# Reordered attention groups, smaller stores of x between the weight loads, and a new order between the expert layers

## The chip, the cores and the metric

The kernel runs on one core of a Trainium2 chip. The metric is the device time of one launch in microseconds (us), lower is better. A core has five engines with queues of their own: PE (TensorE, matrix products), DVE (VectorE), ACT (ScalarE), POOL (GpSimd) and SP (SyncE, which here only issues DMAs). Each runs its instructions in program order, and they wait for one another through semaphores. Sixteen DMA engines move the data.

## The reference

Attention through 32 memory slots for each head, then a dense gated layer ("MoE 1", one expert), then a routed layer with 8 experts ("MoE 2"), all in float32:

```python
# attention: 8 batches x 8 heads, 576 positions, head size 64, 32 slots
a = softmax(phi, axis=slots)                   # exp, divided by the sum + 1e-9
k_m, v_m = a^T k, a^T v                        # 32 x 64 for each head
x = softmax(q k_m^T / 8) v_m                   # 4608 tokens x 512

# MoE 1: 4608 x 512 -> 2048 -> 512
h = x @ w_in
x2 = (h * sigmoid(1.702 * h)) @ w_out

# MoE 2: each token goes to one of 8 experts, 512 -> 1024 -> 512
e = argmax(x2 @ w_gate)
out = prob[e] * sigmoid(x2 @ w_output_gate)[e] * (relu(x2 @ w1[e]) @ w2[e])
```

## The kernel before

**Attention (stage A).** The 64 heads are worked on in 16 groups of 4 heads (g = 0 to 15, `NG` = 16), two groups to a batch. For each group SP loads phi (288 KB), k and v together (1152 KB) and q (576 KB) into triple buffers (`phT`, `kvm`, `qT`); a load into a buffer waits until the group that used it last has been read. The steps of group g, with the line of the kernel before and its tile:

- DVE takes the maximum of phi (`phi_in`, L1162, `csum<-phT`); ACT the exponential (`exp_phi`, L897, `aT`).
- PE transposes it (`a_transposes`, L636 and L639, `ps<-ident,aT`); ACT copies it to SBUF (`a_out`, L907, `am`).
- PE forms k_m and v_m (L653 and L658, `ps<-kvm,am`); ACT scales them with the inverse sums (`kv_scale`, L916, `kvs`); POOL lays v_m out in blocks (`v_blocks`, L1584, `vbd`).
- PE transposes k_m (L668), ACT copies it (`k_out`, L923, `kmT`), and PE forms the scores (L681, `ps<-qT,kmT`).
- DVE transposes the scores (L1173), takes the row maxima (L1175) and subtracts them (L1177, `sc<-sc,scs`); ACT takes the exponential (`exp_scores`, L901); DVE sums and inverts (`inverses`, L1184, L1188, L1190); POOL multiplies by the inverse (`normalize`, L1576); DVE transposes back (`attn_out`, L1196, `pT`).
- PE multiplies by v_m in two halves (`out_half`, L628, `ps<-pT,vbd`); ACT copies the halves out (`x_out`, L933) into `keep` (batches 0 to 6) or `xo` (batch 7).

These steps are staggered by hand: while PE has group g, the scores of g-1 and the outputs of g-3 are worked on. `group(g)` of each engine's program writes that order out; nothing reorders it. `warm_up` (L691) is a product of zeros that nothing reads.

**MoE 1 (stage B).** x is handled in 9 tiles of 512 tokens, each number split into a high and a low part (`xs`: high by a cast, low by a subtraction), so that each float32 product is made of three fast ones. A tile has 16 steps f: `mm1` (L717, 12 matmuls, x by w_in), the gate `g_step` on ACT and DVE (sigmoid L988, product L1237, high part L992, low part L1239), then `mm2` (L750, 12 matmuls, by w_out). In the first tile the weights come too: SP loads 32 chunks of 256 KB (four of them during the attention) (`load_w`) into four raw buffers, and POOL splits each into high and low (`split_w` L1555 and L1557, `split_w_in` L1564 and L1566), which `mm1` and `mm2` wait for through `s_wlo`. W shares memory with `keep`, so POOL may write its second half (steps f = 8 to 15 of w_in and of w_out) only after the x kept there is stored to DRAM (`store_kept`, `kept_stored`). The first tile's first steps are written between the last attention products by hand:

```python
            out_half(NG - 3, 0)
            mm1(0, 0)
            out_half(NG - 3, 1)
            out_half(NG - 2, 0)
            mm1(0, 1)
            out_half(NG - 2, 1)
            for i in range(2):
                out_half(NG - 1, i, (6, 4)[i])
            mm1(0, 2)
```

**MoE 2 (stage C).** Records of 128 tokens (blocks i) are loaded in the order of experts. PE does `block_h` (L791, `ps<-W,cx`) and `block_y` (L820, `ps<-W,chT`), two blocks apart; `dve_x_t`, `act_x_hi` and `dve_x_lo` prepare a block's x (`cxT`, `cx`), `act_relu` and `dve_relu` the two halves of the hidden layer, `act_h_move` moves it with four DMAs, and `dve_h_t`, `act_h_hi` and `dve_h_lo` (L1361, L1053, L1374) transpose and split it (`chT`). Between the stages lie the transposition of the last tile (L849), its logits (L760), the routing of its tokens (`route1`, `route2`) and the tables of blocks on DVE. Six blocks (0 to 5) are written out by hand before the loop starts.

## Time and profile before

| what | value |
|---|---|
| time, three runs | 1333.48 us median (1333.1 to 1334.02) |
| the profiled execution | 1334.72 us, span 1333.0 us |
| PE busy | 1309.6 us, 98% of the span |
| DVE, ACT, POOL busy | 629.7, 388.3, 548.4 us |
| granted PE clock, mean | 0.995 of full |
| DMA share, each 10 us from 10 to 120 us | 0.94 to 1.03 of the time of 16 engines |

The span is the time from the first instruction to the last of one core in one profiled execution; the execution's own time has 1.72 us more around it. An engine is busy while an instruction of it runs; a group's idle time is what the engine stood still just before it, with what ended the wait.

### The profile page before, as it was taken

Reading aid. Unit: us, or ns where it says so; the run is one execution under the profiler, and the core shown is the slowest. Engines: PE = TensorE matmul, PEld = TensorE weight load, DVE = VectorE, ACT = ScalarE, POOL = GpSimd, SP = SyncE. Lnnn points to the kernel's source line nnn. Section 1 sums busy time; section 2 is a strip of 40 time slices with the busy share of each in tenths; the row PEclk is TensorE's granted clock in tenths of the full one; section 3 lists DMA queues with packets and bytes.
Section 4 is the critical chain, followed back from the end, with each engine's and each line's share of the span. In section 5 each row is a group of like instructions: output and inputs, shape, how many; then the busy total and the mean of one; then the engine's idle time right before and its main releaser. Section 6 shows DMA issues by size and latency. Waiting matters only on the chain.

```text
span 1333.0 us, 23549 instructions
## 1 busy us (share of the span) xinstructions
PE 1309.6 (98%) x6872; PEld 1053.5 (79%) x6873; DVE 629.7 (47%) x1291; ACT 388.3 (29%) x725; POOL 548.4 (41%) x649
## 2 busy tenths in 40 slices
PE   7999999999999999999999999999999999999998
PEld 3447888888888888888888888887788888888886
DVE  5893343434433434334434344347555555555553
ACT  4663232222222322222222222223322222222221
POOL 2567944444433434334334343412443242433332
PEclk8999999999999999999999999999999999999999
DMA  9997456575465554654655646647873789549882
GB/s 380 416 405 278 127 201 192 194 194 199 159 180 194 166 178 169 189 174 172 179 185 174 180 170 184 199 159 232 256 206 101 221 238 258 166 128 257 249 247 71
DMA packets 153418, 274.18 MB, mean 206 GB/s; under 512 B 17363, under 2 KB 54612, under 8 KB 150804
## 3 DMA queue, kind: packets, MB, share of 16 engines
q1 hardware_dynamic: 96676, 203.21, 45.2%
q10 hardware_dynamic: 43728, 38.55, 11.8%
q0 software_dynamic: 12960, 31.72, 7.7%
q8 instruction: 31, 0.51, 0.2%
q14 instruction: 23, 0.19, 0.0%
HBM read 144.92 MB, written 100.45 MB: 184 GB/s over the span
## 4 chain that ended last, share of the span: by engine, by line
PE 92%; DVE 3%; DMA 2%; issue 1%; ACT 1%; ACTq 0%; POOL 0%; SPq 0%; POOLq 0%
PE ps L717 29%; PE ps L750 29%; PE ps L820 16%; PE ps L791 15%; DMA phT<-in_phi 2%; PE ps L760 1%; PE ps L628 1%; DVE sc L1173 1%; DVE scs L1175 1%; DVE scs L1184 0%; PE ps L681 0%; ACTq L1046 0%; PE ps L653 0%; DVE sc L1177 0%; DMA cq<-ch 0%
## 5 line engine op out<-in xcount | busy, mean ns | idle before, releaser
L717 PE MATMUL ps<-xs,W 128*128 (+1 forms) x1728 | 417.5, 390 | 0.0
L750 PE MATMUL ps<-W,gs 128*128 128x512 f32 x1728 | 415.0, 389 | 0.1
L717 PEld LDWEIGHTS ps<-xs,W 128*128 128x128 f32 x1728 | 322.9, 188 | 69.7 <-issue 3.1
L750 PEld LDWEIGHTS ps<-W,gs 128*128 128x128 f32 x1728 | 324.2, 188 | 67.8 <-DVE gs L1239 0.5
L1237 DVE TENSOR_TENSOR gate<-ps,gate 128x512 f32<-128x512 f32 x144 | 99.5, 691 | 369.9 <-ACT gate L988 369.9
L988 ACT ACTIVATE gate<-ps 128x512 f32<-128x512 f32 x144 | 86.1, 598 | 467.8 <-PE ps L717 467.3
L820 PE MATMUL ps<-W,chT 128*128 (+1 forms) x936 | 218.3, 389 | 1.5 <-DVE chT L1374 1.5
L791 PE MATMUL ps<-W,cx 128*128 (+1 forms) x936 | 218.5, 389 | 0.4 <-issue 0.4
L1617 POOL CAST whi<-raw 128x512 fp32r<-128x512 f32 x128 | 83.1, 649 | 328.2 <-DMA raw<-in_moe_w 328.2
L820 PEld LDWEIGHTS ps<-W,chT 128*128 128x128 f32 x936 | 175.6, 188 | 38.8 <-issue 2.3
L791 PEld LDWEIGHTS ps<-W,cx 128*128 128x128 f32 x936 | 175.5, 188 | 37.3 <-issue 1.0
L1619 POOL TENSOR_TENSOR raw<-raw,whi 128x512 f32<-128x512 f32 x128 | 171.7, 1341 | 22.4 <-POOL whi L1617 21.1
L383 POOL DMA_DIRECT2D crec<-record_scratch x160 | 90.0, 563 | 187.3 <-DMA out<-cy,cmeta 117.1
L1239 DVE TENSOR_TENSOR gs<-gate,gs 128x512 fp32r<-128x512 f32 x144 | 117.5, 816 | 99.7 <-ACT gs L992 99.7
L992 ACT CAST gs<-gate 128x512 fp32r<-128x512 f32 x144 | 89.4, 621 | 111.3 <-DVE gate L1237 109.1
L1053 ACT CAST chT<-cqT 128x512 fp32r<-128x512 f32 x41 | 25.2, 620 | 201.2 <-issue 152.8
L1625 POOL DMA_INDIRECT record_scratch<-rec,posi x36 | 36.0, 1000 | 99.8 <-DVE posi L1303 90.5
L1676 POOL DMA_INDIRECT out<-cy,cmeta x39 | 42.0, 1078 | 76.2 <-ACT cy L1061 69.0
L1338 DVE TENSOR_TENSOR cx<-cxT,cx 128x512 fp32r<-128x512 f32 x40 | 43.6, 1090 | 58.5 <-ACT cx L1021 56.8
L1374 DVE TENSOR_TENSOR chT<-cqT,chT 128x512 fp32r<-128x512 f32 x78 | 53.2, 691 | 38.0 <-ACT chT L1053 36.7
L1352 DVE TENSOR_SCALAR ch<-ps 128x512 f32<-128x512 f32 x37 | 25.5, 690 | 68.0 <-PE ps L791 67.8
L1361 DVE STREAM_TRANSPOSE cqT<-cq 128x512 f32<-128x512 f32 x78 | 50.6, 686 | 12.6 <-DMA cq<-ch 10.8
(159 smaller groups left out, 779.9 us busy)
## 6 DMA issues: line engine op xcount, KB each, us to landing
W<-expert_scratch SPq DMA_DIRECT2D x24, 2048.0 KB, 11.2
raw<-in_moe_w SPq DMA_DIRECT2D x128, 256.0 KB, 2.8
expert_scratch<-whi SPq DMA_DIRECT2D x128, 256.0 KB, 2.7
expert_scratch<-raw SPq DMA_DIRECT2D x128, 256.0 KB, 3.0
cq<-ch ACTq DMA_DIRECT2D x156, 128.0 KB, 3.8
kvm<-in_kv SPq DMA_DIRECT2D x15, 1152.0 KB, 9.9
crec<-record_scratch POOLq DMA_DIRECT2D x160, 64.0 KB, 3.4
qT<-in_q SPq DMA_DIRECT2D x16, 576.0 KB, 8.2
```

The lines of the kernel that those rows point to most:

```text
L383: eng.dma_start(crec[b * M:(b + 1) * M, r % 3], rows[:, b * P:(b + 1) * P].rearrange("(h n) d -> n h d", n=M)).then_inc(loaded, 16)
L717: mm = pe.matmul(ps[:, f % 2, :], W[:, col:col + P], xs[:, bass.ds(x0 + (x_lo * K1 + c) * T, T)], start=(c == 0 and w_lo + x_lo == 0), sto ...
L750: mm = pe.matmul(ps[:, 2 + s, :], gs[:, f % 2, g_lo, s * P:(s + 1) * P], w_out_sb[:, f, w_lo, :], start=(f == 0 and g_lo + w_lo == 0), sto ...
L791: mm = pe.matmul(ps[:, 3 * u + j, :], cx[:, u, x_lo, c, :], W[:, bass.ds(col, 512)], start=(c == 0 and x_lo + w_lo == 0), stop=(c == K1 - ...
L820: mm = pe.matmul(ps[:, 5 + r % 2, :], chT[:, r % 2, h_lo, c, :], W[:, bass.ds(col, DM)], start=(c == 0 and h_lo + w_lo == 0), stop=(c == C ...
L988: act.activation(gate[:, f % 2, :], ps[:, f % 2, :], ACT.Sigmoid, scale=QTOK).then_inc(b_sig, 1)
L992: act.copy(gs[:, f % 2, 0, :], gate[:, f % 2, :]).then_inc(b_ghi, 1)
L1237: dve.tensor_tensor(gate[:, f % 2, :], ps[:, f % 2, :], gate[:, f % 2, :], ALU.mult).then_inc(b_g, 1)
L1239: dve.tensor_tensor(gs[:, f % 2, 1, :], gate[:, f % 2, :], gs[:, f % 2, 0, :].bitcast(F32), ALU.subtract).then_inc(b_glo, 1)
L1374: dve.tensor_tensor(by_h(1, j), cqT[:, j * 512:(j + 1) * 512].rearrange("p (h c n) -> p h c n", h=2, n=M), by_h(0, j).bitcast(F32), ALU.su ...
L1617: pool.tensor_copy(whi[:, u, :], raw[:, u, :]).then_inc(e_hi, 1)
L1619: pool.tensor_tensor(raw[:, u, :], raw[:, u, :], whi[:, u, :].bitcast(F32), ALU.subtract).then_inc(e_lo, 1)
```

## The change

It has three parts.

1. Attention. The subtraction of the row maxima moves from DVE to POOL for groups 0 to 14 (`less_max`). phi is loaded, and its maximum and exponential are taken, one group earlier. On PE the transposition of phi for the next group moves behind that of k, in two parts, the k/v product goes to another PSUM bank, and two more warm-up products stand before group 0. ACT's order in a group changes. At the end of the stage a first sigmoid stands ahead of the last exponential of the scores, POOL makes both parts of the first two pieces of x, one more `mm1` comes ahead of the first `mm2`, and splits of weights come in another order.
2. Stores of x. In place of two stores of five batches and two for each of batches 5 and 6, the first half of the features of batches 0 to 4 is stored in one piece, and all else in pieces of 576 KB, each after one load of a weight chunk. POOL waits for the first half of the features only before w_in's steps 8 to 11, and for the rest before steps 12 to 15 and w_out's steps 8 and on.
3. Between the expert layers. PE has the transposition of the last x2 tile between the two halves of `block_h` for block 0. DVE has `route1` ahead of `dve_x_lo(2, 0)`, and `dve_x_t(3, 3)` ahead of two `dve_scale`, and `dve_relu(3, 1)` ahead of `dve_x_t(5, 5)`. ACT has `act_x_hi(3, 1)` ahead of `act_y(1, 1)`. Two casts (the high part of block 5's x and of block 3's hidden layer) move from ACT to DVE. POOL loads block 6's records ahead of `scatter_out(1, 1)`.

The core of the diff:

```diff
@@ SP, loads of the attention
             load_phi(0)
             sp.dma_start(ident[:], cst["ident"]).then_inc(s_cst, 16)
+            load_phi(1)
             load_q(0)
+            load_phi(2)
             for g in range(1, NG):
-                load_phi(g)
                 load_kv(g)
                 load_q(g)
+                if g + 2 < NG:
+                    load_phi(g + 2)
@@ SP, first tile (load_w_out(f), load_w_in(c, k): one chunk each)
-            for c in range(2):
-                load_w(K1 + 2 * c, w_out_v[c])
-                load_w(K1 + 2 * c + 1, w_in_part(c, 1))
-            store_kept(0, FIRST, s_xfirst)
+            load_w_out(0)
+            load_w_out(1)
+            load_w_in(0, 1)
+            load_w_in(1, 1)
+            store_kept(0, FIRST, 0, s_xu0)
...
+                    load_w_in(2, 1)
+                    store_kept(FIRST, 1, 0, s_xu0)
+                    load_w_in(3, 1)
+                    store_kept(FIRST + 1, 1, 0, s_xu0)
+                    load_w_out(2)
+                    store_kept(0, 1, 1, s_x10)
+                    load_w_out(3)
+                    store_kept(1, 1, 1, s_x11)
+                    load_w_out(4)
...
@@ PE
+            def group(g):
+                kv_product(g)
+                if g >= 3:
+                    out_half(g - 3, 0)
+                k_transposes(g)
+                if g + 1 < NG:
+                    a_main(g + 1)
+                    pe.wait_ge(s_kmT, g + 1)
+                    a_rest(g + 1)
+                scores(g)
                 if g >= 3:
                     out_half(g - 3, 1)
...
             out_half(NG - 3, 0)
             mm1(0, 0)
             out_half(NG - 3, 1)
+            mm1(0, 1)
             out_half(NG - 2, 0)
-            mm1(0, 1)
             out_half(NG - 2, 1)
+            mm1(0, 2)
             for i in range(2):
                 out_half(NG - 1, i, (6, 4)[i])
-            mm1(0, 2)
+            mm1(0, 3)
...
-            for j in range(2):
-                block_h_half(0, j, 0, 0)
+            block_h_half(0, 0, 0, 0)
             last_x2_transpose(NT - 1)
+            block_h_half(0, 1, 0, 0)
             last_logits(NT - 1)
@@ ACT, group(g)
+                kv_scale(g, u)
                 if g >= 4:
                     x_out(g - 4, 1)
+                k_out(g)
+                if g == 0:
+                    exp_phi(1)
+                if g >= 3:
+                    x_out(g - 3, 0)
+                if g + 1 < NG:
+                    a_out(g + 1)
                 if g:
                     exp_scores(g - 1, 1 - u)
+                if g + 2 < NG:
+                    exp_phi(g + 2)
@@ ACT, first tile
                     if first and f == 2:
-                        stage_a_done(act)
+                        act.wait_ge(s_xst, 16)
@@ DVE, group(g)
-                if g + 1 < NG:
-                    phi_in(g + 1)
-                inverses(g, u, g >= 2, True)
-                if g:
-                    less_max(g - 1, 1 - u)
+                scores_in(g - 1, (g - 1) % 2)
+                inverses(g - 2 if g >= 2 else None, g + 1 if g + 1 < NG else None)
+                scores_max(g - 1, (g - 1) % 2)
+                if g + 2 < NG:
+                    phi_in(g + 2)
                 if g >= 2:
                     attn_out(g - 2)
@@ DVE, blocks 3 to 5
+            dve_x_t(3, 3)
             dve_scale(1, 1)
             dve_scale(2, 2)
-            dve_x_t(3, 3)
...
+            dve_relu(3, 1)
             dve_x_t(5, 5)
-            dve_relu(3, 1)
-
+            dve_x_hi(5, 1)
             dve_x_lo(5, 1)
             dve_scale(5, 5)
             dve_relu(4, 0)
             dve_h_t(3, 1)
+            dve_h_hi(3, 1)
             dve_h_lo(3, 1)
@@ POOL
             for g in range(NG):
+                if g - 1 in QUARTER:
+                    c = QUARTER.index(g - 1)
+                    split_w_in(c, c, 0)
+                if g >= NG - 2:
+                    x_first(g - (NG - 2))
                 if g >= 2:
                     normalize(g - 2, g % 2)
+                if g:
+                    less_max(g - 1, 1 - g % 2)
                 v_blocks(g, g % 4)
...
+            split_w(n_out(0), 0)
+            normalize(NG - 2, 0)
```

**PE, from the start of the program to the k/v product of group 1.** L691 and L744 are the warm-up, `ident,aT` the transposition of phi, `kvm,am` the k/v product, `ident,kvs` the transposition of k, `qT,kmT` the scores. Before:

```order
L691 MATMUL ps<-padrec 128x512
L653 MATMUL ps<-kvm,am 32x128 x16
L658 MATMUL ps<-kvm,am 32x128 x4
L636 MATMUL ps<-ident,aT 128x128 x4
L639 MATMUL ps<-ident,aT 64x64 x2
L668 MATMUL ps<-ident,kvs 64x128 x2
L681 MATMUL ps<-qT,kmT 32x288 x8
L653 MATMUL ps<-kvm,am 32x128 x16
```

Now:

```order
L744 MATMUL ps<-padrec 128x512 x3
L695 MATMUL ps<-kvm,am 32x128 x16
L700 MATMUL ps<-kvm,am 32x128 x4
L709 MATMUL ps<-ident,kvs 64x128 x2
L723 MATMUL ps<-qT,kmT 32x288 x8
L676 MATMUL ps<-ident,aT 128x128 x4
L682 MATMUL ps<-ident,aT 64x64 x2
L695 MATMUL ps<-kvm,am 32x128 x16
```

Two warm-up products are added, and group 1's transposition has moved from before group 0's scores to behind them.

**DVE, one group in the middle of the attention.** `csum<-phT` is the maximum of phi, `sc<-ps` the transposition of the scores, `scs<-sc` a row sum or a row maximum, `pT<-sc` the transposition back. Before:

```order
L1162 TENSOR_REDUCE csum<-phT 128x1
L1184 TENSOR_REDUCE scs<-sc 128x18
L1188 TENSOR_SCALAR scs<-scs 128x19
L1190 RECIPROCAL scs<-scs 128x19
L1173 STREAM_TRANSPOSE sc<-ps 128x288 x2
L1175 TENSOR_REDUCE scs<-sc 128x18
L1177 TENSOR_TENSOR sc<-sc,scs 128x576
L1196 STREAM_TRANSPOSE pT<-sc 128x576
```

Now:

```order
L1247 STREAM_TRANSPOSE sc<-ps 128x288 x2
L1261 TENSOR_REDUCE scs<-sc 128x18
L1265 TENSOR_SCALAR scs<-scs 128x19
L1267 RECIPROCAL scs<-scs 128x19
L1252 TENSOR_REDUCE scs<-sc 128x18
L1236 TENSOR_REDUCE csum<-phT 128x1
L1274 STREAM_TRANSPOSE pT<-sc 128x576
```

The subtraction is gone, and the transposition of the scores stands first.

**ACT, from the last copies of kept x to the store of the last x.** `gate<-ps` is the sigmoid, `sc<-sc` the exponential of the last group's scores, `gs<-gate` the high part of the gate. Before:

```order
L901 ACTIVATE sc<-sc 128x576
L933 COPY keep<-ps 128x2x288
L933 COPY xo<-ps 128x2x288
L988 ACT_TABLE_LOAD
L988 ACTIVATE gate<-ps 128x512
L992 CAST gs<-gate 128x512
L933 COPY xo<-ps 128x2x288 x3
L938 DMA xT_scratch<-xo 128x4x576
```

Now:

```order
L1048 ACT_TABLE_LOAD
L1048 ACTIVATE gate<-ps 128x512
L962 ACT_TABLE_LOAD
L962 ACTIVATE sc<-sc 128x576
L994 COPY keep<-ps 128x2x288
L1055 CAST gs<-gate 128x512
L1048 ACT_TABLE_LOAD
L1048 ACTIVATE gate<-ps 128x512
L994 COPY xo<-ps 128x2x288 x2
L1055 CAST gs<-gate 128x512
L994 COPY xo<-ps 128x2x288 x2
L999 DMA xT_scratch<-xo 128x4x576
```

The exponential now stands between two sigmoids, and each change of function has a table load of its own: three in place of one.

## Rows read from the trace of the kernel before

**Rows 1.** Page, part 1: busy time of each engine, share of the span, instructions

```profile
PE 1309.6 (98%) x6872; PEld 1053.5 (79%) x6873; DVE 629.7 (47%) x1291; ACT 388.3 (29%) x725; POOL 548.4 (41%) x649
```

**Rows 2.** Windows: length, busy time of PE, PEld, DVE, ACT, POOL, clock, DMA, GB/s

```profile
79.54:84.44 4.90, 4.68 (x79) 2.57 (x77) 4.76 (x10) 3.58 (x9) 2.12 (x2) 1.00 1.02 419
93.42:96.83 3.41, 3.36 (x24) 1.42 (x25) 3.31 (x7) 1.17 (x2) 1.61 (x3) 0.50 0.99 419
120.00:140.00 20.00, 20.00 (x90) 16.56 (x89) 6.57 (x8) 4.26 (x7) 19.20 (x20) 1.00 0.43 121
```

**Rows 3.** Timeline of SP and DMA issues of 76.0 to 79.3 us (last column: landing)

```profile
76.15 0.33 SPq L457 DMA_DIRECT2D kvm<-in_kv  x1
...
kvm<-in_kv SPq DMA_DIRECT2D x1, 1152.0 KB, 9.4
qT<-in_q SPq DMA_DIRECT2D x1, 576.0 KB, 7.9
```

**Rows 4.** Timeline of PE, start: start, length, engine, line, operation, count

```profile
9.79 2.07 PE L691 MATMUL ps<-padrec 128*128 128x512 f32 x2
11.79 1.94 PE L653 MATMUL ps<-kvm,am 128*32 128x128 f32 x32
...
25.32 1.08 PE L653 MATMUL ps<-kvm,am 128*32 128x128 f32 x32
```

**Rows 5.** Timelines of DVE and POOL: the subtraction, and POOL's operation of that shape

```profile
81.42 0.76 DVE L1177 TENSOR_TENSOR sc<-sc,scs 128x576 f32<-128x576 f32 x1
...
84.87 1.16 POOL L1576 TENSOR_TENSOR sc<-sc,scs 128x576 f32<-128x576 f32 x1 [2.38 <-DVE scs L1190]
```

**Rows 6.** Timeline of PE, end of the attention

```profile
89.33 1.08 PE L653 MATMUL ps<-kvm,am 128*32 128x128 f32 x32
...
91.54 0.44 PE L668 MATMUL ps<-ident,kvs 128*64 128x128 f32 x4 [0.77 <-ACT kvs L916]
...
93.47 1.21 PE L681 MATMUL ps<-qT,kmT 64*32 64x288 f32 x16 [0.80 <-ACT kmT L923]
94.61 2.29 PE L628 MATMUL ps<-pT,vbd 64*128 64x288 f32 x8
96.83 3.03 PE L717 MATMUL ps<-xs,W 128*128 128x512 f32 x12
99.79 1.24 PE L628 MATMUL ps<-pT,vbd 64*128 64x288 f32 x8
...
105.65 0.76 PE L628 MATMUL ps<-pT,vbd 64*128 64x288 f32 x4 [0.51 <-ACT xo L933]
...
109.20 5.60 PE L750 MATMUL ps<-W,gs 128*128 128x512 f32 x24
```

**Rows 7.** Timeline of ACT, the table load and the first sigmoid

```profile
101.13 0.65 ACT L933 COPY xo<-ps 128x576 f32<-128x576 f32 x1
101.79 1.28 ACT L988 ACT_TABLE_LOAD   x1
103.09 0.60 ACT L988 ACTIVATE gate<-ps 128x512 f32<-128x512 f32 x1
```

**Rows 8.** Timeline of DVE, a small operation beside POOL's subtractions of 87.35 to 89.86

```profile
88.61 1.28 DVE L1188 TENSOR_SCALAR scs<-scs 128x19 f32<-128x19 f32 x1
```

**Rows 9.** Timeline of POOL, the wait in the first tile's splits

```profile
119.87 1.11 POOL L1555 CAST W<-raw 128x512 fp32r<-128x512 f32 x1 [4.46 <-DMA raw<-in_moe_w_out]
```

**Rows 10.** Timeline of PE, idle times between the expert layers

```profile
904.63 1.08 PE L760 MATMUL ps<-x2x,wg 128*32 128x128 f32 x32 [0.83 <-ACT x2x L1103]
...
923.28 11.22 PE L820 MATMUL ps<-W,chT 128*128 128x512 f32 x48 [0.80 <-DVE chT L1374]
934.92 16.60 PE L791 MATMUL ps<-W,cx 128*128 x72 [0.42 <-issue]
952.25 5.72 PE L820 MATMUL ps<-W,chT 128*128 x24 [0.73 <-DVE chT L1374]
```

**Rows 11.** Timeline of DVE, transposition of block 5's x

```profile
941.14 0.71 DVE L1333 STREAM_TRANSPOSE cxT<-crec 128x512 f32<-128x512 f32 x1 [2.70 <-DMA cmeta<-record_scratch]
```

More of the change, by code:

```diff
@@ new lines, in sp_tile @@
+                    sp.dma_start(stage[0], cst["before"]).then_inc(s_cst2, 16)
+                    sp.dma_start(stage[1], gates).then_inc(s_cst2, 16)
+                    sp.wait_ge(b_setup, 1)
+                    sp.dma_start(padrec[:].bitcast(I32)[:, DM + NE + 1:DM + NE + 2], cst["padtoken"]).then_inc(b_cst, 16)
+                    load_w_out(8)
+                    load_w_out(9)
+                    for c in range(K1):
+                        load_w_in(c, 3)
+                    for f in range(10, C1):
+                        load_w_out(f)
@@ L695, in _ @@
             pe.wait_ge(s_cst, 16)
-            a_transposes(0)
-            warm_up(1)
-            for g in range(NG):
+            a_main(0)
+            a_rest(0)
+            warm_up(3)
+            kv_product(0)
+            k_transposes(0)
+            scores(0)
+            a_main(1)
+            a_rest(1)
+            for g in range(1, NG):
                 group(g)
@@ L825, in pe_tile @@
                 for f in range(STEPS):
-                    if not first or f >= 3:
+                    if not first or f >= 4:
                         mm1(t, f)
-                    if f:
+                    if first and f == 4:
+                        mm2(t, f - 2)
+                    if f and not (first and f == 3):
                         mm2(t, f - 1)
-                    elif not first:
+                    if f == 0 and not first:
                         mm2(t - 1, C1 - 1)
@@ L1073, in act_tile @@
                         load_x(t + 1)
-                    if not first or f:
+                    if not first or f >= 2:
                         g_step(t, f)
                     if first and f == 2:
-                        stage_a_done(act)
+                        act.wait_ge(s_xst, 16)
+                    if first and f == STEPS - 1:
+                        kept_stored(act)
                     if not first:
@@ L1088, in act_tile @@
                         x_hi(t + 1, f - 11)
-            g_step(0, 0)
-            x_out(NG - 2, 1)
-            x_out(NG - 1, 0, 6)
-            x_out(NG - 1, 1, 4)
+            g_sigmoid(0, 0)
+            exp_scores(NG - 1, 1)
+            x_out(NG - 3, 1)
+            g_hi(0, 0)
+            g_sigmoid(0, 1)
+            for i in range(2):
+                x_out(NG - 2, i)
+            g_hi(0, 1)
+            for i in range(2):
+                x_out(NG - 1, i, (6, 4)[i])
             store_last()
```

265 lines of the change are left out of this document (149 added, 116 removed).

## The prediction

> **What bounds the kernel now.** I read the page first. PE is busy for 1309.6 of 1333.0 us [rows 1]: the products of the three stages stand on it almost without a gap, and nothing in the change removes a product. Time can only come from PE's idle time and from the attention, where PE's instructions wait for others or run below their best. So I went on with the windows of the attention, and with the timeline of PE wherever idle time stands before a row.
>
> In the attention's second half one group takes 4.9 us. In a window of that length DVE is busy for 4.76 of 4.90 us, PE for 4.68, ACT for 3.58, POOL for 2.12, and the DMA engines all the time at 419 GB/s [rows 2]. Two bounds lie on top of each other: DVE's work for a group, and the 2016 KB that a group loads (2.06 MB by 0.42 MB/us is 4.9 us). Which came last is seen in the last group: its k and v were issued at 76.15 and landed 9.4 us later, at 85.6 [rows 3], but PE began their product only at 89.33 [rows 6]. The compute engines are 3.8 us behind the data. That lag can be won; the landing itself can't, since the bytes up to it are the same in both kernels.
>
> Behind that product PE does what is left of the attention and three `mm1` until 109.20, and from there it has no idle time of over 0.12 us until 904 us (the timeline shows none). In these 19.9 us it is idle for 0.77, 0.80 and 0.51 us, and it runs at half clock from 93.42 to 96.83 (granted 0.50, its lower level of 1.2 GHz), after the two idle times; four halves of attention output take 2.29 us there against 1.24 us later [rows 2, 6]. Between the expert layers four idle times stand ahead of PE's products: 0.83, 0.80, 0.42 and 0.73 us, together 2.8 us [rows 10].
>
> **The attention's pace.** The subtraction leaves DVE, 0.76 us [rows 5], so that DVE needs 4.76 - 0.76 = 4.0 us for a group. POOL takes it at the 1.16 us of its own operation of that shape [rows 5]: 2.12 + 1.16 = 3.3 us, and 5.3 us in the four groups in which it also splits a chunk (0.61 and some 1.3 us). These fall into the 1.8 us in which POOL would wait for the inverse sums, so at most 0.5 us of each shows. PE has 4.68 us in a group, less than the loads' 4.9. Its new order leaves the same instructions, and each wait has cover: `kmT`'s copy lies behind the main transposition of phi, `kvs` behind half an output. ACT's 3.58 us are unchanged. So the loads alone set the pace, and compute may run at 4.7 us for as long as it is behind them.
>
> **The start is worse.** The two added warm-up products run at half clock, the first takes 2.07 us and about 1.7 us without its start [rows 4]; they put off the product of group 0 from 11.79 by 3.4 us, which gives 1.0 us back as it then runs at full clock (1.94 against 1.08 us [rows 4]). Group 1's transposition and copy now lie behind the scores of group 0, another 1.4 us. So the compute starts 3.5 to 4 us late: group 3's product moves from 25.32 [rows 4] to about 29. At 4.7 us for each of the next 12 groups the last group's product could begin at 29 + 56 = 85. The loads feel the start too. phi of group 4, which stands ahead of group 3's k and v on SP, waits for the exponential of group 1, which on ACT now stands behind group 0's copy of k, at about 19 us; the loads issued earlier have landed at 19.3, and a load needs about 2 us to begin. That is up to 1.5 us without a transfer, and nothing makes it up in a stage bound by the loads. I take 0.8 us of it, as the present kernel's k and v of group 3 landed late too. The last product then begins at 85.6 + 0.8 + 0.1 = 86.5 in place of 89.33: **2.8 us won**. Bounds: 85.7 (nothing lost) and 89 (the pace is 4.9 to 5.0 us, since PE's waits aren't all covered).
>
> **The tail.** From that product to 109.20 PE needs 19.9 us, less 2.1 us of idle time and 1.5 us of half clock, so 16.3 us of dense work [rows 6]. It now has a fourth `mm1` ahead of the first `mm2`, the same work in another place, 2.7 us; the corresponding point of the kernel before is 109.20 + 2.7 = 111.9. Still idle will be about 0.4 us before the last scores, whose copy of k has no other work over it. Walking the new order through with X as the last product's start: the last scores end at X + 3.6, the first `mm1` runs from X + 5.0 to 7.7. Then ACT loads the sigmoid's table ahead of time, does the sigmoid (X + 8.4), loads the exponential's table (1.28 us [rows 7]), and does the exponential (X + 10.4). DVE sums, inverts, multiplies (0.8 to 1.6 us) and transposes: `pT` of the last group is there at X + 14.1 to 15.5. PE asks for it at X + 14.9, behind the third `mm1`. The third load, 1.28 us, lies ahead of the sigmoid for the fourth `mm1`, whose own wait (for DVE's product of step 1) ends at X + 15.4 to 16.4, against a need at X + 16.1. Both are near a stall; I allow 0.4 us. So the corresponding point is X + 16.3 + 2.7 + 0.8 = X + 19.8 = 106.3 against 111.9: 5.6 us, of which **2.8 us are the tail's**.
>
> In rows 7 the table load takes 1.28 us, begins when the copy before it has ended (101.13 + 0.65), and the sigmoid follows it at once. The Trainium skill (ScalarE: Activation LUTs, What ACT_TABLE_LOAD costs) puts a change of set at about 2.66 us, a load of 1.28 and a drain of 1.38. No drain is seen in rows 7, so the trace doesn't agree; by that rule the last `pT` would come 1.4 us later. What a stall there would cost is the third rival below.
>
> A small DVE operation can also be held up by POOL: the one at 88.61 took 1.28 us until POOL's second subtraction ended, and 0.17 us elsewhere [rows 8]. In the tail POOL splits without a pause, and DVE's sums with 1e-9 and inversions stand in the chain to `pT`; that is the upper end of X + 15.5. The Trainium skill (SBUF — State Buffer, Who interferes with whom) says the same of this operation and excludes reductions; the steady groups keep theirs, so their pace stands.
>
> **Stores and weights.** The four chunks of w_in for steps 4 to 7 are wanted at about X + 24, earlier than now by 5.6 us. POOL splits a chunk in 2.0 us (19.20 us busy for 10 in 20 us [rows 2]). It ends w_out 0 and the fourth of them, six chunks and a `normalize`, at about X + 18.7, if they have landed. The big store of 2880 KB is 7 us of transfers, the two pieces of 576 KB 1.4 us each; the last of the four chunks lands at about X + 14. The cover is 5 us. POOL waits 4.46 us for a store and a chunk at 119.87 now [rows 9] and PE feels nothing; the new pieces come no later. Cost: 0. If the cover is gone, each microsecond of delay is one of the whole.
>
> **Between the layers.** The 0.83 us before the logits is the wait for copies of the transposed tile; the second half of block 0 now covers it, and all of routing comes 0.8 us earlier. The 0.80 us at 923.28 comes from block 1's four moves on ACT and stays. The 0.42 us before block 3 waits for its low part on DVE; `dve_x_t(3, 3)` goes ahead of six small operations, 0.9 us: gone. The 0.73 us before block 3's second product comes from DVE's half of its relu, queued behind a transposition that waited 2.70 us for block 5's records until 941.14 [rows 11]; it now stands ahead, and the casts take 1.1 and 0.7 us on DVE, which has that much idle time there. Gone too. **2.0 us won**, between 0.8 (only the logits) and 2.8.
>
> **Sum.** 2.8 + 2.8 + 2.0 = 7.6 us. Against the profiled execution (span 1333.0, time 1334.72) that is a span of 1325.4 and a time of 1327.1; that execution lies 1.2 us above the median, so against 1333.48 the time is 1325.9 us.
>
> **Rivals.**
> - *The attention's pace doesn't change* (12%). PE's chain of waits, not DVE, would set it. For it speaks that PE is busy for 4.68 of 4.90 us. The 12 groups from 25.32 to 89.33 took 5.33 us each now; the late start then moves X to 29 + 64 = 93, and the end by 93 + 19.8 - 111.9 = +0.9, less 2.0: 1332.4, no change. Against it: DVE shows no idle time in these groups, PE does.
> - *The pace improves by half* (15%): X = 89, time 1328.4.
> - *The tail stalls on the last exponential* (10%). With 1.4 us more on each switch and POOL's hold on DVE, PE waits 2 to 3 us before the last outputs: 1328 to 1329.
> - *Slower* (4%): the first tile's weights. POOL has 1.16 us more in each group and casts two pieces of x; its last `normalize` and w_in's chunks, loaded only after earlier ones are split, come late, and step 4 waits. It decides from where the last chunk is split 5.5 + 7.6 = 13 us later than I work out: at X + 32 it gives 1333.5, at X + 36 1337.5. Against it: POOL's present pace.
> - The forecast, 1323.5 to 1327.5: 59%.
>
> Faster by over 0.2% (2.7 us, about what a measurement of this kernel can tell) is below 1330.8: 0.87. Within it: 0.09. Slower: 0.04. The range goes from 1323.0 (nothing lost at the start, 2.8 us between the layers) to 1329.5, which takes in the half-improved pace and the stalled tail.
>
> **What would show it.** The last k/v product at 86 to 87 us, not 89.3; the pace of DVE below 4.2 us busy in a group; three table loads of 1.28 us, with less than 1 us idle before the last outputs; no idle time on PE from then to the logits; idle times of 0.83, 0.42 and 0.73 us gone and that of 0.80 us kept. Wrong would be: k/v products that follow one another by more than 4.9 us where no chunk is loaded, a DMA share well under 1 from 19 to 25 us, or a wait of step 4 for W.

## The result, and the profile after

The changed kernel takes 1329.81 us (median of 12 runs, 1328.08 to 1331.56) against 1333.1 us for the kernel before beside it (12 runs, 1332.13 to 1334.56); the ratio is 0.9972, with a 95% interval of 0.9965 to 0.9979. A repeat of the comparison gave 1329.18 us and 0.9966 (0.9954 to 0.9979). So it is faster, by 3.3 to 3.8 us; the forecast was 7.6 us, and its time, 1325.9 us, lies 3.9 us below the median; the upper end of its range, 1329.5 us, lies between the two medians. Why only half of it came is what the rest is about.

Page of the changed kernel, one line of part 1 (busy time) and one of part 4 (the chain that ended last):

```profile
PE 1306.9 (98%) x6876; PEld 1052.2 (79%) x6877; DVE 624.0 (47%) x1281; ACT 389.5 (29%) x722; POOL 564.8 (43%) x666
...
PE 93%; DMA 4%; DVE 1%; ACT 1%; issue 0%; POOL 0%; ACTq 0%; SPq 0%; POOLq 0%; DVEq 0%
```

The two profiled executions, cut at the same events of PE (in us; each mark is the start of a PE row; the fourth `mm1` is ahead of the mark of the tail only after the change, so its 2.72 us are added to 109.20 before):

| stretch | before | after | won | forecast |
|---|---|---|---|---|
| start to the last k/v product | 89.33 | 86.59 | 2.74 | 2.8 |
| to the first `mm2` (before: and one `mm1`) | 22.59 | 20.79 | 1.80 | 2.8 |
| to block 0 of the expert layers | 784.53 | 784.53 | 0.00 | 0 |
| to block 3's second product | 55.80 | 54.45 | 1.35 | 2.0 |
| to the end of the span | 380.73 | 380.67 | 0.06 | 0 |

The sum is 5.95 us of span (1332.98 less 1327.03). The medians differ by only 3.3: the profiled execution of before took 1334.72 us, 1.6 above the median of its 12 runs, and that of after 1328.66, 1.2 below its own. A term read from one pair of executions can be far off: the tail's 1.80 becomes 0.25 beside another execution of the old attention (experiment 1).

**The attention.** Windows of the changed kernel (columns as in rows 2), a group of the second half and the start:

```profile
10.00:20.00 10.00, 8.21 (x114) 4.19 (x113) 2.25 (x8) 3.24 (x8) 0.45 (x1) 0.91 1.02 423
...
77.16:81.99 4.83, 4.67 (x76) 2.56 (x76) 3.93 (x9) 3.63 (x9) 3.32 (x5) 1.00 1.03 425
```

Beside the window 79.54:84.44 of [rows 2], DVE has 3.93 us of work in place of 4.76, POOL 3.32 in place of 2.12. The DMA share never falls, at the start either. Timeline of PE after, to be read against [rows 6]:

```profile
77.16 1.08 PE L695 MATMUL ps<-kvm,am 128*32 128x128 f32 x32 [0.21 <-DMA kvm<-in_kv]
...
81.99 1.08 PE L695 MATMUL ps<-kvm,am 128*32 128x128 f32 x32 [0.16 <-DMA kvm<-in_kv]
...
86.59 1.08 PE L695 MATMUL ps<-kvm,am 128*32 128x128 f32 x32
...
89.44 0.72 PE L723 MATMUL ps<-qT,kmT 64*32 64x288 f32 x16 [0.36 <-ACT kmT L984]
...
91.41 0.96 PE L776 MATMUL ps<-xs,W 128*128 128x512 f32 x3
```

The k/v product's releaser is now the load itself. In groups 6 to 14 (from 41.10 us on) it begins 0.04 or 0.05 us after its k and v have landed, where before it began 3.7 to 4.8 us after. The last group is an exception: its k and v landed at 86.14, and PE, which from 81.99 on shows no idle time, came to their product 0.45 us later.

**The tail.** PE, and under it DVE, of the changed kernel:

```profile
102.37 1.24 PE L668 MATMUL ps<-pT,vbd 64*128 64x288 f32 x8 [0.16 <-DVE pT L1274]
104.52 3.02 PE L776 MATMUL ps<-xs,W 128*128 128x512 f32 x12 [0.91 <-DVE gate L1306]
107.38 0.84 PE L808 MATMUL ps<-W,gs 128*128 128x512 f32 x3
```

```profile
101.53 0.78 DVE L1274 STREAM_TRANSPOSE pT<-sc 128x576 f32<-128x576 f32 x1
102.24 1.63 DVE L1311 TENSOR_TENSOR gs<-gate,gs 128x512 fp32r<-128x512 f32 x1
103.79 0.68 DVE L1306 TENSOR_TENSOR gate<-ps,gate 128x512 f32<-128x512 f32 x1
```

The 0.91 us before the fourth `mm1` are new. It waits for DVE's product of step 1 (L1306), which stands behind the low part of step 0 (L1311); that one took 1.63 us, and 0.69 us where POOL left it alone. ACT's tables, in the same execution:

```profile
92.78 1.28 ACT L1048 ACT_TABLE_LOAD   x1
94.48 0.60 ACT L1048 ACTIVATE gate<-ps 128x512 f32<-128x512 f32 x1 [0.42 <-PE ps L776]
95.10 1.28 ACT L962 ACT_TABLE_LOAD   x1
96.39 0.69 ACT L962 ACTIVATE sc<-sc 128x576 f32<-128x576 f32 x1
...
99.11 1.28 ACT L1048 ACT_TABLE_LOAD   x1
100.41 0.60 ACT L1048 ACTIVATE gate<-ps 128x512 f32<-128x512 f32 x1
```

Each load takes 1.28 us. The second and the third begin 0.02 us after the instruction before them has ended, and the function follows at once; behind the first, the sigmoid waits 0.42 us for PE's product. So the trace agrees with the load that the Trainium skill states (ScalarE: Activation LUTs, What ACT_TABLE_LOAD costs), and not with the drain that it adds.

**The weights.** The longest wait of POOL's splits for a chunk before 125 us, at [rows 9]'s place (a second one, 0.95 us, stands at 122.65):

```profile
117.22 0.61 POOL L1656 CAST W<-raw 128x512 fp32r<-128x512 f32 x1 [2.88 <-DMA raw<-in_moe_w_out]
```

PE has no idle time of over 0.12 us from 107.38 to 904 us.

**Between the layers.** PE, and under it ACT and DVE, of the changed kernel, against [rows 10]:

```profile
903.18 8.45 PE L849 MATMUL ps<-W,cx 128*128 128x512 f32 x36
...
918.50 11.15 PE L878 MATMUL ps<-W,chT 128*128 128x512 f32 x48 [1.43 <-DVE chT L1473]
929.92 16.60 PE L849 MATMUL ps<-W,cx 128*128 x72 [0.27 <-issue]
946.36 4.01 PE L878 MATMUL ps<-W,chT 128*128 x17
```

```profile
913.12 3.18 ACTq L1113 DMA_DIRECT2D cq<-ch  x4
916.34 1.14 ACT L1120 CAST chT<-cqT 128x512 fp32r<-128x512 f32 x2 [3.29 <-issue]
```

```profile
917.06 1.29 DVE L1473 TENSOR_TENSOR chT<-cqT,chT 128x512 fp32r<-128x512 f32 x2 [1.37 <-ACT chT L1120]
```

The 0.83 and 0.73 us are gone, 0.42 has become 0.27, and 0.80 has grown to 1.43. What stands ahead of block 3's low part on DVE is now the transposition of its x, and that waits for the block's records:

```profile
926.75 0.71 DVE L1426 STREAM_TRANSPOSE cxT<-crec 128x512 f32<-128x512 f32 x1 [0.63 <-DMA cmeta<-record_scratch]
```

### The profile page after: what moved, and what is told of

Read it like the earlier page. It is cut to its first block, busy times and chain, and to the rows that moved or that the text cites. A ratio compares the mean times of both kernels' runs of the same rounds, so it can differ in the third digit from the quotient of the medians.

```text
span 1327.0 us, 23583 instructions
## 1 busy us (share of the span) xinstructions
PE 1306.9 (98%) x6876; PEld 1052.2 (79%) x6877; DVE 624.0 (47%) x1281; ACT 389.5 (29%) x722; POOL 564.8 (43%) x666
## 4 chain that ended last, share of the span: by engine, by line
PE 93%; DMA 4%; DVE 1%; ACT 1%; issue 0%; POOL 0%; ACTq 0%; SPq 0%; POOLq 0%; DVEq 0%
PE ps L808 29%; PE ps L776 29%; PE ps L849 16%; PE ps L878 16%; DMA kvm<-in_kv 3%; PE ps L818 1%; PE ps L695 1%; DMA phT<-in_phi 0%; PE ps L676 0%; PE ps L744 0%; PE ps L668 0%; ACTq L1113 0%; POOL sc L1677 0%; ACT aT L958 0%; PE ps L709 0%
## 5 line engine op out<-in xcount | busy, mean ns | idle before, releaser
L1306 DVE TENSOR_TENSOR gate<-ps,gate 128x512 f32<-128x512 f32 x144 | 99.6, 692 | 361.7 <-ACT gate L1048 361.4
L1311 DVE TENSOR_TENSOR gs<-gate,gs 128x512 fp32r<-128x512 f32 x144 | 117.1, 813 | 102.0 <-ACT gs L1055 102.0
```

The costliest lines, as they stand in the source:

```text
L1306: dve.tensor_tensor(gate[:, f % 2, :], ps[:, f % 2, :], gate[:, f % 2, :], ALU.mult).then_inc(b_g, 1)
L1311: dve.tensor_tensor(gs[:, f % 2, 1, :], gate[:, f % 2, :], gs[:, f % 2, 0, :].bitcast(F32), ALU.subtract).then_inc(b_glo, 1)
```

## The experiments

Each is the kernel named, with the edit shown. "Pace" is the distance of two k/v products, X the start of the last one. The time is the median, the ratio that to the kernel before beside it, with its 95% interval. Where a profiled execution is compared, it is one execution.

**1. The last part alone** (before, with the new order between the expert layers). Edit, at its core:

```diff
@@ PE, DVE, ACT, POOL of stages B and C: as part 3 of the change
-            for j in range(2):
-                block_h_half(0, j, 0, 0)
+            block_h_half(0, 0, 0, 0)
             last_x2_transpose(NT - 1)
+            block_h_half(0, 1, 0, 0)
...
+            dve_x_t(3, 3)
             dve_scale(1, 1)
             dve_scale(2, 2)
-            dve_x_t(3, 3)
...
```

> The kernel before with the third part alone (order and casts between the expert layers). By the two profiles the stretch from block 0's product to block 3's second product is 1.35 us shorter: theory A expects 1.0 to 1.5 us less than the kernel before, with the idle times of 0.83 and 0.73 us gone and that before block 1's second product kept at 0.8. My prediction had 2.0. Rival: the gap before block 1's second product grows as in the changed kernel (1.43), as it is caused by routing coming earlier; then 0.7 us.

Measured: 1331.03 us (11 runs), ratio 0.9990 (0.9981 to 0.9999). From block 0 to block 3's second product 54.18 us against 55.80: 1.6 won, by the ratio 1.3. Here too the 0.80 us grew, to 1.48, as the rival said; the other three idle times are gone. This kernel has the attention of before untouched, so its profile is a second execution of it. PE, timeline, to be laid beside [rows 6]:

```profile
89.08 1.08 PE L653 MATMUL ps<-kvm,am 128*32 128x128 f32 x32
...
93.22 0.72 PE L681 MATMUL ps<-qT,kmT 64*32 64x288 f32 x16 [0.80 <-ACT kmT L923]
93.86 1.24 PE L628 MATMUL ps<-pT,vbd 64*128 64x288 f32 x8
95.04 1.20 PE L717 MATMUL ps<-xs,W 128*128 128x512 f32 x4
```

The idle times of 0.77 and 0.80 us are the same, but the half clock behind them is not there: the outputs take 1.24 us, not 2.29, and from X to the first `mm1` are 5.96 us, not 7.50. The 1.5 us of half clock belong to the one execution that was profiled before: the kernel before with smaller loads (experiment 4) has the same idle times too, and 5.96 us as well. From X to the end of the tail this execution needs 21.04 us (18.32 and one `mm1`), the changed kernel 20.79: by this pair the new order of the tail wins 0.25 us, not 2.8.

The same profile shows what holds the old attention. Issues of SP from 73.5 to 77 us with their time to landing, and the timeline of SP and of DVE:

```profile
phT<-in_phi SPq DMA_DIRECT2D x1, 288.0 KB, 8.3
...
74.28 0.43 SPq L452 DMA_DIRECT2D phT<-in_phi  x1
...
82.62 0.75 DVE L1160 TENSOR_REDUCE csum<-phT 128x1 f32<-128x576 f32 x1
```

phi of the last group, issued at 74.28, lands 8.3 us later, at 82.6; DVE's maximum of it begins at 82.62, and the product 6.46 us behind that.

**2. The subtraction back on DVE** (after, without `less_max` on POOL):

```diff
@@ DVE, group(g), behind scores_max
+                dve.wait_ge(s_dv, DVE_A * g)
+                dve.tensor_tensor(by_m((g - 1) % 2), by_m((g - 1) % 2), each_m((g - 1) % 2, 0), ALU.subtract).then_inc(s_mx, 1)
@@ POOL
-                if g:
-                    less_max(g - 1, 1 - g % 2)
```

> The changed kernel with the subtraction of the maxima back on DVE for all groups. Theory D (DVE's relief is what lets compute follow the loads): DVE has 4.8 us per group again, the last k/v product comes 2 to 3 us later, the time is 2 to 3 us longer than the changed kernel's. Rival (the new order of PE, ACT and of phi is what won): DVE's 4.8 us are still under the loads' 4.9, the last product stays within 0.5 us of 86.6, and the time within 0.7 us. As the lag at the start is 3 us at group 3, and the loads give 0.1 us per group and 0.6 us per weight chunk, I expect the last product at 87 to 88, and 1 us longer.

Measured: 1333.71 us (11 runs), ratio 1.0005 (0.9996 to 1.0014), 4.5 us above the changed kernel and all of the gain lost, more than either theory had. X is 90.62. DVE and PE in one group:

```profile
79.47 1.21 DVE L1287 TENSOR_TENSOR sc<-sc,scs 128x576 f32<-128x576 f32 x1
80.60 0.74 DVE L1236 TENSOR_REDUCE csum<-phT 128x1 f32<-128x576 f32 x1
81.27 0.76 DVE L1274 STREAM_TRANSPOSE pT<-sc 128x576 f32<-128x576 f32 x1
```

```profile
82.08 0.76 PE L668 MATMUL ps<-pT,vbd 64*128 64x288 f32 x4 [0.64 <-DVE pT L1274]
```

The subtraction costs 1.21 us there (0.76 in [rows 5]), DVE is busy for 5.09 us of each 5.30, and PE waits 0.64 us for `pT` in each group. The new order alone is worse than the old.

**3. The subtraction on POOL, in the old order** (before, plus `less_max` on POOL for all groups but the last, nothing else; the function itself is left out here).

```diff
@@ DVE
-                wait(dve, s_dv, DVE_A * g + 3)
-                dve.tensor_tensor(by_m(u), by_m(u), each_m(u, 0), ALU.subtract).then_inc(s_mx, 1)
+                if g == NG - 1:
+                    wait(dve, s_dv, DVE_A * g + 3)
+                    dve.tensor_tensor(by_m(u), by_m(u), each_m(u, 0), ALU.subtract).then_inc(s_mx, 1)
@@ POOL, behind normalize(g - 2, g % 2)
+                if g:
+                    less_max(g - 1, 1 - g % 2)
```

> The kernel before with one edit: POOL takes the subtraction of the maxima of every group but the last, and nothing else changes (order of PE and ACT as before). If DVE's load alone had set the old pace (4.74 of 4.88 us busy), the last k/v product comes as in the changed kernel, at 85.5 to 87 us, and the time falls by 2 to 3 us. If the old order's chain of waits sets it (the exponential now comes 0.4 us later behind POOL's slower operation, and on ACT and PE the next group stands behind it), the product stays at 88.5 to 90 and the time within 0.1%. I lean to the second, 60 to 40: so the new order and the new engine each do nothing alone.

Measured: 1332.72 us (11 runs), ratio 0.9999 (0.9990 to 1.0008); X is 89.51. DVE has 4.08 us of work in a group now, 0.7 less than before, and nothing is won. Window of one group, DVE and PE:

```profile
79.94:84.68 4.74, 4.67 (x78) 2.56 (x76) 4.08 (x9) 3.58 (x9) 2.73 (x4) 1.00 1.01 417
```

```profile
77.52 0.75 DVE L1162 TENSOR_REDUCE csum<-phT 128x1 f32<-128x576 f32 x1 [0.39 <-DMA phT<-in_phi]
```

```profile
89.51 1.08 PE L653 MATMUL ps<-kvm,am 128*32 128x128 f32 x32
```

With less to do DVE only waits, for phi. The last product comes 7.1 us after phi's landing in place of 6.5, and no group from 4 on takes less than 6.9: POOL's subtraction in the chain takes 1.16 us where DVE's took 0.76. So neither the new engine nor the new order wins alone; only together do they. Which parts of the new order are needed (phi's earlier load, PE's order, ACT's) was not tried one by one.

**4. Fewer bytes** (q loaded by half from group 3 on, so half of the scores' operand is stale: the output, and the experts' load with it, differ; only the attention is read). In the changed kernel and in the kernel before:

```diff
+                part = QA * D if g < 3 else QA * D // 2
-                sp.dma_start(qT[g % 3][:].rearrange("p c h n -> p (c h n)"), q[g * P:(g + 1) * P, :]).then_inc(s_q[g % 3], 16)
+                sp.dma_start(qT[g % 3][:].rearrange("p c h n -> p (c h n)")[:, 0:part], q[g * P:(g + 1) * P, 0:part]).then_inc(s_q[g % 3], 16)
```

> The changed kernel with only half of q loaded from group 3 on; the other half of the buffer keeps older numbers, so the scores are others. 288 KB less in each of 13 groups, 0.7 us of transfers each. Theory L (in the changed kernel the loads set the pace from group 6 on, each k/v product begins 0.05 us after its landing): the groups now follow one another by the compute's own 4.6 us, and the last product begins at 82 to 83 us in place of 86.6 to 87.2. Rival (another engine is as slow): it moves by less than 1 us.

> The kernel before with the same smaller loads. Its k/v products begin 3.8 us after the landing, so by theory L the loads don't set its pace but DVE's chain does: the groups that now take 4.9 us stay at 4.9, only the four with a weight chunk (5.5 us) may fall to 4.9. The last product moves from 89.1 to no less than 86.5. Rival (the loads are the bound in both): it moves as in the changed kernel, by over 4 us.

Measured, one execution each. Changed kernel: X at 83.98, 2.6 and 3.2 us earlier than in the two profiles of it. Kernel before: X at 84.95, 4.1 to 4.4 earlier. A window of one group of each, the changed kernel first:

```profile
74.78:79.38 4.60, 4.60 (x78) 2.56 (x77) 4.27 (x9) 3.83 (x9) 2.87 (x5) 1.00 0.95 382
```

```profile
75.35:80.12 4.77, 4.67 (x78) 2.56 (x76) 4.63 (x10) 3.58 (x9) 2.00 (x2) 1.00 0.91 360
```

Both kernels were paced by the loads: the old one moved as the rival said, past the 86.5 that I had set as its limit. Freed of them the new order makes a group in 4.60 us, with PE never idle, and the old one in 4.77. There DVE is behind the loads in the old order: its maximum of phi begins 2.0 and 2.1 us after phi has landed in the last two groups.

**5. One warm-up product** (after).

```diff
-            warm_up(3)
+            warm_up(1)
```

> The changed kernel with one warm-up product before group 0 in place of three. The prediction said that the two added ones put off group 0 and starve the loads by up to 1.5 us. In the profile the loads never stood still (phi of group 4 was issued at 17.0, the load before it landed at 19.3). Theory A: group 0's product begins 1.5 to 2 us earlier, the last one at the same time, since the loads set it: time the same within 0.5 us. Rival 1 (the start costs): 1 us faster. Rival 2 (the warm-ups keep the clock up): without them the clock is 0.5 for one or two more stretches of 3.4 us, the groups run slower there, and the time is the same or up to 1 us longer.

Measured: 1328.75 us (5 runs), ratio 0.9965 (0.9952 to 0.9979). Group 0's product comes at 11.94 in place of 13.50; X does not move. PE at X:

```profile
87.11 1.08 PE L695 MATMUL ps<-kvm,am 128*32 128x128 f32 x32 [1.12 <-DMA kvm<-in_kv]
```

What the start gains, the loads take. In this execution the last k and v landed at 87.06 (86.14 in the first one). The landing moves between executions: in four of the eight profiles with the changed attention and all its loads (the two of the changed kernel and those of experiments 9 and 10) it comes 4.2 us after the one before, in the other four (experiments 5 to 8) 5.7 to 5.8 us after, and PE then waits 1.0 to 1.1 us at X. The order and the times of issue don't make the difference: in experiments 5 and 10 the load was issued at 73.00 and 73.01, the next q landed at 88.35 in both, and k and v landed at 87.06 and 85.38.

**6. The gate's product first** (after; DVE's product of step 1 ahead of the low part of step 0).

```diff
+            g_product(0, 1)
             g_lo(0, 0)
+            g_lo(0, 1)
...
-                    if not first or f:
+                    if not first or f >= 2:
```

> The changed kernel with DVE's product of step 1 ahead of the low part of step 0. In both profiles of the changed kernel PE is idle for 0.91 us before the fourth mm1 and waits for that product, which DVE does behind a low part of 1.63 us. Theory T (this one wait is what the tail lost): the 0.9 us are gone, the first mm2 begins 0.9 us earlier in relation to the last k/v product (20.8 to 19.9 us), the time is 0.9 us shorter. Rival: the low part, now later, holds up the first mm2, and the idle time only moves there.

Measured: 1328.0 us (5 runs), ratio 0.9961 (0.9948 to 0.9975). From the first `mm1` to the first `mm2` 14.74 us against 15.97 and 15.98 in the two profiles of the changed kernel. That overstates it: in experiment 5, without this edit, the same stretch took 14.85. There PE had waited 1.12 us for the last k and v, as it did for 1.09 us here, and DVE had caught up; in experiments 7 and 8, with the same wait, the stretch is 15.10 and 14.99 and the idle time before the fourth `mm1` 0.28 and 0.18 us. So its 0.91 us stand only in executions in which the load doesn't make PE wait at X; the two take each other's place. This run therefore doesn't show what the edit wins; the profile of experiment 10 does.

**7. Block 1's cast on DVE** (after).

```diff
@@ ACT
-            act_h_hi(1, 1)
@@ DVE
+            dve_h_hi(1, 1)
```

> The changed kernel with the high part of block 1's hidden layer cast on DVE, which on ACT stands behind the issue of block 2's four moves. Theory C (PE reaches block 1's second product 0.9 us earlier than before, but that cast stays where it was, so the idle time of 0.8 us grew to 1.1 to 1.4): the idle time before that product is gone; as the tables behind it on DVE come only some 0.6 us earlier, PE's idle time before block 3 grows from 0.3 to 0.5 us to about 1.0; net 0.5 to 0.9 us faster. Rival: what holds it is the landing of block 1's moves, and DVE's cast changes nothing.

Measured: 1329.03 us (5 runs), ratio 0.9966 (0.9952 to 0.9979); block 0 to block 3's second product 54.02 us (54.45 and 54.38 before the edit). PE still waits 1.04 us before block 1's second product, and none before block 3: both parts of theory C failed. DVE there:

```profile
914.65 1.30 DVE L1459 STREAM_TRANSPOSE cqT<-cq 128x512 f32<-128x512 f32 x2 [0.87 <-DVE crec L1568]
915.88 0.46 DVE L1571 TENSOR_REDUCE crec<-crec 1x43 f32<-1x344 f32 x1
916.26 0.49 DVE L1572 TENSOR_REDUCE crec<-crec 1x43 f32<-1x344 f32 x1
916.78 0.76 DVE L1465 CAST chT<-cqT 128x512 fp32r<-128x512 f32 x2
```

The cast no longer waits for ACT's four moves, but two reductions of the block tables now stand ahead of it: one wait took the place of the other.

**8. The stores first** (after; the second half of the features of batches 0 to 4 stored right behind the big store, ahead of the weights of steps 4 to 7 in part and of all later ones).

```diff
@@ SP, behind store_kept(0, FIRST, 0, s_xu0)
+            for b, stored in enumerate((s_x10, s_x11, s_xu1, s_xu1, s_xu1)):
+                store_kept(b, 1, 1, stored)
... (and the five taken out at their old places)
```

> The changed kernel with the five single pieces of x (batches 0 to 4) stored right behind the big store in place of between the loads of W. If the weights of steps 4 to 7 have some 5 us of cover, the 2.9 MB, up to 7 us of transfers ahead of W's chunks, show as POOL's waits and at most 2 us of PE's idle time before 140 us: time +0 to +2 us. If the rival is right that the first tile hangs on the weights, every microsecond shows: +4 to +7 us. I expect +0 to +2.

Measured: 1328.28 us (6 runs), ratio 0.9966 (0.9954 to 0.9978). 2.9 MB now stand ahead of these weights; POOL waits for a chunk at 105.73 us, PE for none, and the time is no longer than the changed kernel's:

```profile
105.73 0.61 POOL L1665 CAST W<-raw 128x512 fp32r<-128x512 f32 x1 [2.88 <-DMA raw<-in_moe_w_in]
```

**9. One table load** (after; ACT's last exponential ahead of the first sigmoid).

```diff
+            exp_scores(NG - 1, 1)
             g_sigmoid(0, 0)
-            exp_scores(NG - 1, 1)
```

> The changed kernel with ACT's last exponential ahead of the first sigmoid, so that ACT changes its table once in place of three times. If the table loads (1.28 us each) held the tail, the last outputs' waits go and the time falls by up to 1 us. If DVE's order before the fourth mm1 holds it, the sigmoid that comes later puts off DVE's products and so that mm1: 0 to +1.5 us. I expect the second.

Measured: 1329.49 us (6 runs), ratio 0.9970 (0.9958 to 0.9982): no difference from the changed kernel. ACT:

```profile
95.76 0.69 ACT L962 ACTIVATE sc<-sc 128x576 f32<-128x576 f32 x1 [3.31 <-DVE sc L1321]
96.46 1.28 ACT L1048 ACT_TABLE_LOAD   x1
```

Two loads (2.56 us) are saved, and ACT waits 3.31 us for DVE's subtraction instead. The order written with three loads costs nothing that these runs show.

**10. Experiments 5, 6 and 7 together.** The edit is the three above.

> The changed kernel with three edits: DVE makes the gate product of step 1 ahead of the low part of step 0, block 1's high cast is on DVE, one warm-up product in place of three. If the idle time before the fourth mm1 (0.91 us) and half of the gap before block 1's second product are what was given back, the time is 1.2 to 1.8 us below the changed kernel's 1329.2 to 1329.8: 1327.4 to 1328.4. If these only shift which wait comes last, it is 1328.5 to 1329.5.

Measured: 1327.89 us (5 runs, 1326.6 to 1329.48), ratio 0.9962 (0.9948 to 0.9975). It is the lowest median, 1.3 to 1.9 us below those of the changed kernel, though the intervals of the ratios overlap, and experiment 6 alone had 1328.0: what the other two edits add doesn't show. PE and DVE in the tail:

```profile
101.61 1.24 PE L668 MATMUL ps<-pT,vbd 64*128 64x288 f32 x8 [0.17 <-DVE pT L1273]
102.78 3.04 PE L776 MATMUL ps<-xs,W 128*128 128x512 f32 x12
105.66 0.62 PE L808 MATMUL ps<-W,gs 128*128 128x512 f32 x2
```

```profile
101.48 0.65 DVE L1305 TENSOR_TENSOR gate<-ps,gate 128x512 f32<-128x512 f32 x1
102.05 2.08 DVE L1310 TENSOR_TENSOR gs<-gate,gs 128x512 fp32r<-128x512 f32 x2
```

Here PE had not waited at X (85.83), as in the changed kernel's profile; an idle time of 0.17 us before the outputs is there as well, and the 0.91 us before the fourth `mm1` are gone. First `mm1` to first `mm2`: 15.02 against 15.97. Block 1's gap stays at 1.05 us.

The changed kernel unaltered, the repeat named at the top, had this expectation:

> The changed kernel once more, for a second profile. In the first one its span was 6.0 us shorter than that of the kernel before, while the medians differ by 3.3 us. Theory A (the shown profile is a lucky one): this profile has a span of 1328 to 1329 us, and the last k/v product or the point where PE becomes dense comes 1 to 2 us later than 86.6 and 107.4. Theory B (the time is lost outside the span): the span is again 1327 and the time still 1329.8.

Measured, besides the times at the top: the profiled execution has a span of 1327.5 us, X is 87.16 and the first `mm2` comes at 107.94, 0.6 us later than in the first profile. That is less than theory A had. Theory B fails too: outside the span are 1.7 us, as in the other two profiles. The larger part of what the two first profiles show too much lies in the one of the kernel before, 1.6 us above its median.

## Why the prediction was half right

**The last k/v product: near in its time, wrong in its reason.** Forecast 86.5, measured 86.59 and 87.16, and 85.83 to 88.38 in the six other profiles with this attention and all its loads; that the first came so near is in part luck. The landing moved by 0.6 us to 86.14 (forecast 0.8), and the start, warm-ups and all, cost nothing that the loads didn't cover (experiment 5). "The compute engines are 3.8 us behind the data" was so; that DVE's 4.76 us of work kept them there was not. Experiment 3 takes 0.7 us of work in each group from DVE and X stays. In the kernel before, DVE's maximum begins 0.02 us after phi has landed in nearly every group, and the product 6.5 us after it: the lag is the length of the chain from phi to the product, less the 2.7 us by which phi lands ahead of k and v. SP now loads phi two groups ahead; the last one lands 6.9 us before its k and v, and the chain no longer shows. The subtraction had to leave DVE because the new order can't bear it there (experiment 2: 0.64 us of waiting in each group), not because it had set the pace. My first rival, that the pace is PE's chain of waits, fell too: it priced 5.33 us a group as compute, and it was the loads' pace (experiment 4).

**The tail: the term that failed.** I took 2.1 us of idle time and 1.5 us of half clock out of it, and allowed 0.8 us. Two faults. The half clock stood in one execution only; the profiles of experiments 1 and 3, with the same order on PE and the same idle time of 0.77 us (the second one 0.80 and 0.36), show full clock there (X to the first `mm1` 5.96 and 5.51 us). A sum made against the profiled execution may contain it, but then it can't be carried to the median, and I subtracted all of 7.6 us from it. And of the 2.1 us of idle time, 1.1 us came (first `mm1` at X + 4.8, not X + 6.0) and 0.9 us were given back before the fourth `mm1`. I had its wait "near a stall", ending at X + 15.4 to 16.4 against a need at X + 16.1; it ended at X + 17.9. PE asked for it at X + 17.0, later than I had it. I had left DVE's order out: the low part of step 0 stands ahead, and it took 1.63 us beside POOL's splits. Experiment 10 shows it: with DVE's product ahead of the low part the 0.91 us are gone, in an execution without a wait at X. The third rival, a stall on the last exponential, didn't come: 0.16 us. (A reading of the rows was off as well, without effect on the sum: the eight matmuls of 2.29 and 1.24 us are two halves of an output, not four.)

**Between the layers: 1.35 for 2.0 us.** 0.83 and 0.73 went as forecast. "The 0.80 us at 923.28 stays" was wrong: PE arrives 0.9 us earlier, while the moment of release hardly moved (26.6 us after block 0's start, 26.8 before), so most of what the moved transposition had won was waited away there. A wait for something that isn't moved grows by what is won ahead of it. Experiment 7 shows that it has two releasers close together, ACT's cast and DVE's order. Nor was the 0.42 us before block 3 "gone": 0.27 and 0.48 us are left in the two profiles, and 1.69 in that of experiment 5, where DVE's transposition, now ahead of the small operations, waited 2.15 us for the block's records.

**Stores and weights: right, nothing.** 0 us at 784.53 us between tail and blocks, and experiment 8 shows that 2.9 MB may go ahead of the weights. The rival "slower" didn't come.

**The sum.** In the profiles of PE's old order without the half clock in the tail (experiments 1 and 3) the last k/v product is at 89.3 us on the mean and block 0 at 894.65 in both. In five profiles with the changed attention and tail (the two, and those of experiments 5, 7 and 8) they are at 87.3 and 891.9. So the product won 2.0 us where 2.8 were forecast, the tail 0.7 for 2.8 (1.5 of the difference is the clock), the layers 1.35 to 1.6 for 2.0 by the two profiles and experiment 1. That is 4.1 to 4.3 us, of which the two ratios show 3.7 and 4.5. The layers' term moves too: 0.4 us in the profile of experiment 5, by the wait for the records, and in that of experiment 9 the stretch is 0.8 us longer than before (56.60 us), with 2.52 us of idle time and 3.4 us at a granted clock of 0.50 behind it.

What stays open: how often the half clock of the tail comes in runs that aren't profiled, and why the last k and v land at 85.4 to 88.3 us. The record has the mean granted clock of each run, without its place: it is 0.996 or less in 20 of 48 runs of the kernel before and in 1 of 18 of the changed one. The five runs of the kernel before at 0.995, as in the profiled one, took 1333.9 us on the mean, and the nine at 0.999 took 1332.8. So the changed kernel runs at half clock less often, and part of the gain may come from that; how much, and whether the median before contains the tail's 1.5 us, isn't shown.

## What to carry to other kernels

An engine that is busy for 97% of a group need not be what sets the group's pace: look at the start of the first instruction that reads a load. Where it begins at the landing in every group, the loads set the pace and the lag behind them is the chain's length. Relieving the busy engine did nothing alone here; what removed the lag was loading the chain's first operand earlier together with a new order and the relief. Before a clock stretch or any idle time of one profiled execution goes into a sum, look whether the median contains it; and where a step is pulled forward, go along the whole queue of each engine that releases it, with the durations that hold beside its neighbours, and carry what is won up to the next fixed release.

## What the hardware showed that I had not expected

The same idle times of 0.77 and 0.80 us were followed by 3.4 us at a granted clock of 0.50, the lower level of 1.2 GHz, in one execution [rows 2, 6] and by none in two others (experiment 1, and the kernel before in experiment 4). DVE's subtraction of two SBUF operands, 128x512, took 0.69 us alone and 1.63 us beside POOL's splits, and that of 128x576 1.21 us beside POOL's `normalize` (experiment 2) against 0.76 [rows 5]; the Trainium skill (SBUF — State Buffer, Who interferes with whom) says that such an instruction, with two inputs in SBUF, contends with POOL's reads, and these rows agree. From 10 to 86 us the changed kernel's DMAs moved 414 GB/s on the mean with a share of 1.02, and those of the kernel before 415 GB/s with 1.01: the loads ran at the same rate in both, and only the compute's lag behind them changed. One load of 1152 KB, issued at the same time among the same others, landed 1.7 us later in one execution than in another (experiments 5 and 10).
